# Attention's weights times values: seven of fifteen key tiles as three fp32r passes over high and low parts

## The reference

```python
scores = scale * np.matmul(q, k.transpose(0, 1, 3, 2))
scores = np.where(causal, -1000000000.0, scores)
a = np.exp(scores - scores.max(-1, keepdims=True))
a /= a.sum(-1, keepdims=True) + 1e-09
local = np.matmul(a, v)
mem_out = np.einsum('bhsd,bhde->bhse', phi(q), M_prev) / mem_norm
out = g * mem_out + (1 - g) * local
```

## Time and profile before

| | |
|---|---|
| Median of 3 runs | 870.16 us (870.12 to 870.6) |
| The profiled execution's own time | 870.0 us |
| Its span in the profile | 868.3 us |
| PE busy | 855.3 us (99%) |
| PEld busy | 755.7 us (87%) |
| DVE, ACT, POOL busy | 492.5, 317.6, 257.3 us |
| Attention | from the start to about 255.7 us |

### The profile page before, as it was taken

One profiled execution on the slowest core, in us unless ns is written; L12 is line 12 of the kernel. 1 busy time (PEld: TensorE's weight loads), 2 busy tenths in 40 slices (PEclk: granted clock), 3 DMA queues, 4 the chain that ended last, 5 costly groups with the idle time before them and its releaser, 6 DMA issues.

```text
span 868.3 us, 13401 instructions
## 1 busy us (share of the span) xinstructions
PE 855.3 (99%) x4966; PEld 755.7 (87%) x4966; DVE 492.5 (57%) x1036; ACT 317.6 (37%) x572; POOL 257.3 (30%) x371
## 2 busy tenths in 40 slices
PE   8999999999999999999999999999999999999998
PEld 7899999999888888888888889999998888888886
DVE  7766666666548865433443344344757655656664
ACT  6656566565432223222322222232243323232322
POOL 5656656565569992000000000000600000000000
PEclk9999999999999999999999999999999999999999
DMA  8665757564403322000000000000210000000000
GB/s 148 149 139 124 162 126 157 131 151 97 118 25 103 112 89 62 1 1 0 1 1 1 0 1 1 1 1 1 89 57 13 12 25 25 24 24 24 13 24 36
DMA packets 86359, 49.27 MB, mean 57 GB/s; under 512 B 65056, under 2 KB 73248, under 8 KB 86304
## 3 DMA queue, kind: packets, MB, share of 16 engines
q1 hardware_dynamic: 83760, 47.94, 22.8%
q10 hardware_dynamic: 2544, 0.59, 0.4%
HBM read 27.28 MB, written 4.72 MB: 37 GB/s over the span
## 4 chain that ended last, share of the span: by engine, by line
PE 89%; DVE 7%; issue 2%; ACT 1%; POOL 0%; POOLq 0%; ACTq 0%
PE ps_h L1265 8%; PE ps_h L1267 8%; PE ps_h L1266 8%; PE ps_y L1280 7%; PE ps_y L1282 7%; PE ps_y L1281 7%; PE ps_v L631 7%; PE ps_hid L1541 4%; PE ps_r L1570 4%; PE ps_s L546 4%; PE ps_hid L1543 4%; PE ps_hid L1542 4%; PE ps_r L1572 4%; PE ps_r L1571 4%; DVE spent L948 3%
## 5 line engine op out<-in xcount | busy, mean ns | idle before, releaser
L1384 DVE TENSOR_TENSOR xT<-xT 128x512 f32<-128x512 f32 (+1 forms) x80 | 60.3, 754 | 133.7 <-ACT xT L1340 133.7
L1265 PE MATMUL ps_h<-x_hi,win 128*128 128x512 f32 (+1 forms) x320 | 117.7, 368 | 0.0
L1267 PE MATMUL ps_h<-x_hi,win 128*128 128x512 f32 (+1 forms) x320 | 117.5, 367 | 0.0
L1282 PE MATMUL ps_y<-g_hi,wout 128*128 128x512 f32 (+1 forms) x320 | 117.5, 367 | 0.0
L1281 PE MATMUL ps_y<-g_lo,wout 128*128 128x512 f32 (+1 forms) x320 | 117.5, 367 | 0.0
L1266 PE MATMUL ps_h<-x_lo,win 128*128 128x512 f32 (+1 forms) x320 | 117.5, 367 | 0.0
L1280 PE MATMUL ps_y<-g_hi,wout 128*128 128x512 f32 (+1 forms) x320 | 117.4, 367 | 0.0
L631 PE MATMUL ps_v<-v_raw,pT 128*128 128x65 f32 (+1 forms) x960 | 107.6, 254 | 1.2 <-DVE t_loc L1046 1.2
L631 PEld LDWEIGHTS ps_v<-v_raw,pT 128*128 128x128 f32 (+1 forms) x960 | 101.3, 173 | 6.9 <-issue 4.7
L948 DVE CUSTOM_DVE_ANT_0 spent<-ps_s,mask 128x576 f32<-128x576 f32 (+4 forms) x160 | 81.6, 539 | 42.4 <-PE ps_s L546 41.6
L767 ACT ACTIVATE pT<-ps_x 128x512 f32<-128x512 f32 (+3 forms) x128 | 64.1, 501 | 94.5 <-PE ps_x L613 93.6
(11 more groups left out here) (164 smaller groups left out, 1685.7 us busy)
## 6 DMA issues: line engine op xcount, KB each, us to landing
stacked<-cut SPq DMA_DIRECT2D x56, 288.0 KB, 5.2
out<-res SPq DMA_DIRECT2D x18, 256.0 KB, 2.0
v_raw<-in_v SPq DMA_DIRECT2D x32, 128.0 KB, 3.2
stage<-in_moe_w_in SPq DMA_DIRECT2D x16, 256.0 KB, 2.7
stage<-in_moe_w_out SPq DMA_DIRECT2D x16, 256.0 KB, 2.6
k_raw<-in_k SPq DMA_DIRECT2D x28, 128.0 KB, 2.5
q_raw<-in_q SPq DMA_DIRECT2D x28, 128.0 KB, 3.6
stage<-in_moe_w_in SPq DMA_DIRECT2D x4, 512.0 KB, 3.8
```

The lines of the kernel that those rows point to most:

```text
L1265: pe.matmul(out, hi, x_hi[:, k, 0:n], start=(k == 0), stop=False)
L1267: ins = pe.matmul(out, lo, x_hi[:, k, 0:n], start=False, stop=(k == KT - 1))
L1282: ins = pe.matmul(out, wout[:, f, LO, w], g_hi[:, r, 0:n], start=False, stop=(f == FT - 1))
L1384: dve.tensor_tensor(r, r, r, ALU.mult).then_inc(square_done, 1)
```

## The change

Of the fifteen products of weights and values of a head, the seven with key tile j = 0 or 1 and a full query tile (t < 4) are done as three fp32r passes: high weights times high values (66 columns), high weights times low values (64 columns), low weights times high values (66 columns). It applies from head 4 (`WHOLE`) to head 31; heads 0 to 3 stay as they were. For this

- ACT writes the high weights `p_hi` (`round_weights`, two instructions a head: 384 columns for j=1 and 512 for j=0),
- DVE writes the low weights `p_lo` (`low_weights`, 384 and 512 columns),
- POOL writes the high and low values `v_cut` of key tiles 0 and 1, once a pair (`cut_values`),
[...]
- PE does `cross(h, 1)` before the first products of head h-1 instead of behind them, and waits there for `p_lo` and `v_cut` too,
- some buffers shrink: `stacked` holds keys and queries of a head next to each other, `fT` and `K1` lose the padding to 640 columns, `t_mem` has two buffers and not three, `least` one, `spent` shares places. The last memory product of a pair has 64 queries instead of 128.

Core of the diff:

```diff
@@ tensor: weigh_values
+                if is_cut(h):
+                    pe.wait_ge(v_lo_done, p - DIRECT + 1)
+                    pe.wait_ge(weights_low, 2 * (h - WHOLE) + 2)
             for t in ts:
+                where = EVEN * t
                 for j in range(t + 1):
                     at, m = p_at[j] + P * (t - j), rows_of[t]
-                    ins = pe.matmul(ps_v[0:m, par, E1 * t:E1 * (t + 1)], pT[par][:, at:at + m],
+                    if is_cut(h) and j < 2 and t < FULL:
+                        part = halves[j].start + P * (t - j)
+                        high = p_hi[par][:, part:part + P]
+                        low = p_lo[par][:, part:part + P]
+                        values = v_cut[h // 2 % 2]
+                        pe.matmul(ps_v[:, par, where:where + EVEN], high, values[:, 0, j, par, :],
+                                  start=(t == 0), stop=False, skip_group_check=True)
+                        pe.matmul(ps_v[:, par, where:where + D], high, values[:, 1, j, par, 0:D],
+                                  start=False, stop=False, skip_group_check=True)
+                        ins = pe.matmul(ps_v[:, par, where:where + EVEN], low, values[:, 0, j, par, :],
+                                        start=False, stop=(j == t), skip_group_check=True)
+                        continue
+                    ins = pe.matmul(ps_v[0:m, par, where:where + E1], pT[par][:, at:at + m],
                                     v_raw[h // 2 % 3][:, j, par, :], start=(t == 0),
@@ tensor: steps
+                if here:
+                    cross(h, 1)
                 if behind:
                     weigh_values(h - 1, (0, 1))
                 if ahead:
                     second_rows(h + 2)
-                if here:
-                    cross(h, 1)
@@ scalar
+        def round_weights(h, j):
+            act.wait_ge(tri_done, h * NT + (1 if j == 1 else 4))
+            act.wait_ge(exped, h * NC + (1 if j == 1 else 3))
+            act.activation(p_hi[h % 2][:, halves[j]], weights_of(h, j), ACT.Copy).then_inc(weights_rounded, 1)
...
                     exp_weights(h, 1)
+                if is_cut(h):
+                    round_weights(h, 1)
...
                     exp_weights(h, 3)
-                    if aside:
-                        aside(3)
+                if is_cut(h):
+                    round_weights(h, 0)
+                if here and aside:
+                    aside(3)
@@ vector
+        def low_weights(h, j):
+            dve.wait_ge(weights_rounded, 2 * (h - WHOLE) + (1 if j == 1 else 2))
+            if h > WHOLE + 1:
+                dve.wait_ge(pv_done, h - 1)
+            dve.tensor_tensor(p_lo[h % 2][:, halves[j]], weights_of(h, j), p_hi[h % 2][:, halves[j]],
+                              ALU.subtract).then_inc(weights_low, 1)
...
+                if is_cut(h - 1):
+                    low_weights(h - 1, 0)
                 if ahead or is_head(h + 1):
                     first_rows(h + 2)
                 if ahead:
                     second_rows(h + 2)
+                if is_cut(h):
+                    low_weights(h, 1)
+                if ahead:
                     third_rows(h + 2)
@@ gpsimd
+        def cut_values(p):
+            both, half = v_raw[p % 3][:, 0:2, :, :], v_cut[p % 2]
+            pool.wait_ge(v_in[p % 3], 16 * Q_DMAS * (p // 3 + 1))
+            need(pool, pv_done, 2 * (p - 2) + 2)
+            pool.tensor_scalar(half[:, 0, :, :, 0:E1], both, 1.0, 1.0, ALU.mult, ALU.mult).then_inc(v_hi_done, 1)
+            pool.wait_ge(v_hi_done, p - DIRECT + 1)
+            pool.tensor_tensor(half[:, 1, :, :, 0:D], both[:, :, :, 0:D], half[:, 0, :, :, 0:D], ALU.subtract).then_inc(v_lo_done, 1)
```

More of the change, by code:

```diff
@@ L117, in attention @@
     SLOTS, LATE = 3, 4
-    Q_HI, Q_LO, K_HI = range(3)
+    K_HI, Q_HI, Q_LO = range(3)
     MEM = 172
@@ L148, in attention @@
                         for places in ((pT[0][:, 0:THREE], all_t_mem[:, 0:THREE]),
-                                       (pT[1][:, 0:THREE], all_t_mem[:, THREE:2 * THREE])))
+                                       (pT[1][:, 0:THREE], all_relu[:, 0:THREE])))
     rm, rl = sb("rm", [P, NT, 2]), sb("rl", [P, 2, NT])
+    halves = {1: slice(0, wide[1] - REST), 0: slice(wide[1] - REST, wide[1] - REST + wide[0] - REST)}
+    p_hi, p_lo = ([sb(f"p_{n}{s}", [P, halves[0].stop], F32R) for s in range(2)] for n in ("hi", "lo"))
+    v_cut = [sb(f"v_cut{s}", [P, 2, 2, 2, EVEN], F32R) for s in range(2)]
     beta_in, inv_gate, inv_rest = (sb(n, [P, H]) for n in ("beta_in", "inv_gate", "inv_rest"))
@@ L219, in words, with is_cut, weights_of, both @@
         return view.bitcast(F32)
+    def is_cut(h):
+        return WHOLE <= h < HEADS
+    def weights_of(h, j):
+        return pT[h % 2][:, p_at[j]:p_at[j] + wide[j] - REST]
+    def both(view):
+        return view.rearrange("p (two s) -> p two s", two=2)
     def stacks_sent(p):
@@ L321, in gpsimd @@
                            base=0, pattern=[[-1, P]], channel_multiplier=1).then_inc(built, 1)
[L322 to L326, removed]
+        pool.memset(words(stacked[:, :, 2 * S:S + W]), 0.0).then_inc(cleared, 1)
+        pool.memset(least[:, :], 0.0).then_inc(cleared, 1)
         for s in range(3):
@@ L418, in steps @@
                     features(pr + 1)
+                if not even and is_pair(pr + 1):
+                    cut_values(pr + 1)
         double(first_k[1], k_in[1])
@@ L536, in memory @@
             for t in range(NT):
-                ins = pe.matmul(ps_t[:, MEM * t:MEM * t + 2 * E1], fT[p % 2][:, P * t:P * (t + 1)],
+                m = rows_of[t]
+                ins = pe.matmul(ps_t[0:m, MEM * t:MEM * t + 2 * E1], fT[p % 2][:, P * t:P * t + m],
                                 mz[:, p, :], start=True, stop=True)
@@ L574, in first_rows @@
             if is_head(h - 1):
-                ins = pe.transpose(ps_s[:, NEG_AT:NEG_AT + P], least[(h - 1) % 2][:, :], ident[:, :])
+                ins = pe.transpose(ps_s[:, NEG_AT:NEG_AT + P], least[:, :], ident[:, :])
             ins.then_inc(scored, 1)
@@ L611, in cross @@
                 out = ps_x[0:rows_of[j], c % 2, at:at + hi - lo]
-                pe.matmul(out, stacked[:, a, 1, some], stacked[:, a, 0, lo:hi], start=True, stop=False)
+                pe.matmul(out, stacked[:, a, some], stacked[:, a, S + lo:S + hi], start=True, stop=False)
                 ins = pe.matmul(out, K1[0:kept, p % LATE, par, some], Q1[0:kept, p % SLOTS, par, lo:hi],
@@ L809, in put @@
                 act.wait_ge(kT_turned, p + 1)
-                place, source = stacked[MINE[half], to, 1, 0:S], keys_psum(p)[MINE[half], 0:S]
+                place, source = stacked[MINE[half], to, 0:S], keys_psum(p)[MINE[half], 0:S]
             elif what[:-1] == "k_moved":
                 act.wait_ge(swapped_turned, K_SWAPPED[p])
-                place, source = stacked[MINE[1 - half], to, 1, 0:S], \
+                place, source = stacked[MINE[1 - half], to, 0:S], \
                     ps_x[:, :, :].rearrange("p two n -> p (two n)")[MINE[1 - half], 0:S]
@@ L816, in put @@
                 act.wait_ge(qT_turned, p + 1)
-                place, source = stacked[MINE[0], to, 0, 0:S], ps_t[MINE[0], 0:S]
+                place, source = stacked[MINE[0], to, S:2 * S], ps_t[MINE[0], 0:S]
             elif what == "q_own1":
@@ L822, in put @@
                 act.wait_ge(swapped_turned, Q_SWAPPED[p])
-                place, source = stacked[MINE[0], to, 0, 0:S], swapped_psum(p)[MINE[0], 0:S]
+                place, source = stacked[MINE[0], to, S:2 * S], swapped_psum(p)[MINE[0], 0:S]
             else:
@@ L946, in row_maximum @@
             n, r = keys[t], min(P, S - P * t)
-            at, at_row = sum(keys[:t]), SHIFT[h % 2].start + t
+            at, at_row = SPENT_AT[t], SHIFT[h % 2].start + t
             return dve.tensor_tensor_reduce(spent[:, at:at + n], ps_s[:, S_AT[t]:S_AT[t] + n],
                                             mask[:, FULL * P + r - n:FULL * P + r], -1.0, HUGE,
-                                            ALU.add, ALU.min, least[h % 2][:, at_row:at_row + 1])
+                                            ALU.add, ALU.min, least[:, at_row:at_row + 1])
         def first_rows(h):
@@ L1035, in scale_local @@
             kt = place(p)[1]
-            got = ps_v[:, :, 0:NT * E1].rearrange("p two (t e) -> p two t e", e=E1)
+            got = ps_v[:, :, 0:NT * EVEN].rearrange("p two (t e) -> p two t e", e=EVEN)
             dve.wait_ge(pv_done, 2 * p + 2)
```

56 lines of the change are left out of this document (31 added, 25 removed).

## The result

The changed kernel takes 902.95 us, the median of four runs (897.95 to 903.34), against 870.38 (870.12 to 870.82) of the kernel before on the same chip: 1.036 times as long [1.0324, 1.0397]. It is slower, as forecast, but 9.7 us above the forecast and 4 above the range's upper end. Its mean granted clock, 1.0 before, was 0.989, 0.994, 0.987 and 0.987 in the four runs; the quickest of them, 897.95, is the one at 0.994.

The account below looks back on a forecast made before the run. PE's list, busy 99% at full clock, was taken to bound the kernel, weight loads setting the changed products' pace. 870.0 + 21.6 (loads) + 0 (odd step) + 1.5 (end of attention) = 893.1, as median 893.3 us; range 886.5 to 898.8.

Parts of the forecast that it names:

- 196 products, one load more each: Seven products a head, heads 4 to 31: three loads, 0.333 us, replace 0.223; +21.6 us (18.0 to 23.9).
- Order of PE, buffers: `cross(h, 1)` moved ahead shrinks PE's wait for the row maximum, at best 2.8 us back; smaller buffers cost about nothing.
- Waits for `p_lo` and other feeding: Odd steps: PE waits for `p_lo` only if DVE's subtraction is slowed; taken as 0, at worst 2.8 us more.
- Wait at the end of attention: Last head's products wait for `p_lo`, which stands behind the first MLP's four `x_lo` on DVE: +1.5 us (1.1 to 1.9).
- The step that failed: Opening step: PE, busy 99% at full clock, bounds the kernel; attention grows by PE's list and its new waits.
- The load as the price of a pass: Each fp32r pass in attention costs one weight load, 0.111 us, whatever its 66 or 64 columns need; three cost 0.333.
- Rival 1: Fast loads: the passes' loads come at 0.058 us, a product costs 0.174 instead of 0.223; 862 us; 3%.
- rival 2: One load serves the two passes with the same high weights, so a product keeps its old price; 871.7 us; 2%.
- rival 3: Passes come closer than loads, 0.09 us apart: +9.2 us, 881 us; 4%.
- The rule on fast loads: Loads of 128 columns and non-FP32 type speed up by themselves; fp32r could count, giving the sum the other sign.
- The wait in an odd step: PE's wait for DVE's row maximum: PE comes 0.92 us later, DVE 0.69; taken as 0, 2.8 us either way.
- rival 4: DVE sets the pace: 512-column subtractions take 1.11 us, PE waits 0.42 in each of 28 heads; +11.8, 905 us; 8%.

Follow-up runs that it names:

- e1: The changed kernel with every product of weights and values in fp32 again, no parts made or waited for; new order and buffers stay: 865.98 us.
- e8: e2 with the last head's `p_lo` put ahead of the fourth `x_lo` on DVE: 891.27 us.
- e2: The changed kernel with each pass's moving columns read twice (132, 128, 132), the second copy going to PSUM columns nobody reads: 896.87 us.
- e5: The changed kernel without the second pass (high weights times low values), so two fp32r loads a product: 880.83 us.
- e7: The changed kernel with `p_hi`, `p_lo` and `v_cut` made and waited for, but the seven products of each head left in fp32: 881.14 us.
- e4: The changed kernel with only heads 4 to 27 in three passes, heads 28 to 31 left in fp32: 886.55 us.
- e9: The changed kernel with the last head's `p_lo` ahead of the fourth `x_lo` on DVE, passes as they were: 900.22 us.
- e10: e7 with the last head's `p_lo` ahead of the fourth `x_lo` on DVE: 877.87 us.

## Why the prediction was wrong

The measured terms are below. The loads and the wait at the end are read from traces. The others are differences of medians, less these two where it says so; the column therefore adds up by construction. A term that compares runs of different groups is uncertain by about half a microsecond.

| Term | Predicted | Measured |
|---|---|---|
| 196 products, one load more each | +21.6 | +21.8 (196 x 0.111 from the loads) |
| Order of PE, buffers | 0 (with the next) | -4.4 (e1 against before) |
| Waits for `p_lo` and other feeding | 0 | +3.5 (e8 - e1 - 21.8) |
| Wait at the end of attention | +1.5 | +2.2 (2.63 in e2 less 0.44 in e8) |
| Clock behind that wait | none | +3.4 (e2 - e8 - 2.2) |
| Clock under the narrow passes | none | +6.1 (after - e2) |
| Sum over before | +23.1 | +32.6 |

**The step that failed** is the first one: "PE is busy 99% of the span at a granted clock of full speed". That was read from before and carried over to the changed kernel as if it were a property of the core. The last sentence of the prediction named the case (wrong "if the granted clock leaves full speed"), but no rival had it and no end of the range paid for it. It is worth 3.4 + 6.1 = 9.5 us of the 9.7 missed, about what the half-clock stretches of the two traces can cost: 20.5 / 2 = 10.2 in the changed kernel. Rows for a warning were there: the pace of these products was already that of their loads, and the change makes three load and matmul records of two, at about the same 65 columns for each load. The other misses (+0.2, -4.4, +3.5, +0.7) cancel, by luck.

**The load as the price of a pass** was right, in size too: 0.11 apart, 21.8 against 21.6. Rival 1 (862), rival 2 (871.7) and rival 3 (881) need closer loads or one for two passes; neither is in the trace, and e5 and e7 agree. The rule on fast loads that the prediction takes from the Trainium skill, TensorE: Matmul & The Clock Gate, section Weight-path perf modes — Fast Weight Load (FWL) and DoubleRow, isn't borne out for the fp32r loads here: they last 195 to 197 ns each, fp32 ones 191.

**The wait in an odd step** came out near its 0 because two terms nearly cancel, which is luck: -4.4 for the order and +3.5 for the feeding. The order alone gives 14.69 - 14.44 = 0.25 us a pair, and 4.4 in all, above the 2.8 I had as the best case. What DVE newly does takes most of it back: over e1 a pair of e8 (16.09) is 1.65 longer, of which 14 x 0.111 = 1.55 are loads, so 0.10 a pair or 1.4 us are waits; the other 2.1 of the 3.5 lie outside the steady pairs and were not taken apart. A pair of 16.13 us fits the forecast 16.2.

**DVE as the pace (rival 4, 905)** came near the time, and for the wrong reason. DVE has slack in every pair and PE none; its subtraction of 512 columns took 0.68 or 0.82 us and not 1.11 in the steady part. DVE's work was under-priced all the same, 3.6 us a pair against 2.5, as 384 columns took 0.68 and 1.45 and not 0.554; the slack took it. ACT and POOL came out as sized (0.63 and 0.52 us; 1.1 a pair against 1.3). That the nearest forecast number was that of a wrong mechanism shows why the time alone doesn't settle one.

**The end of attention** was right as a mechanism, with DVE's `p_lo` behind the `x_lo` as releaser, and too small: 2.2 against 1.5 (1.1 to 1.9). The last `x_lo` ended 1.79 us after its start, with 1.09 for `p_lo` behind it; a late `x_hi` of ACT, 1.27 us of waiting, came on top. The `x_lo` was priced at 0.69 to 1.11: POOL was cutting the MLP's weights beside it (L1281, to 277.90), and `x_lo` ended 0.55 us after that. What a wait there does to the clock behind it was not in the term.

**Open:** what amount of work on the array decides, and over what time; why the clock falls in some runs and not in others of the same kernel (e4 and e8, one of four each), which also leaves the first fall of 6.8 us partly to chance; and whether values as the stationary operand, fewer loads for the same products, would save the change. None was tried.

## What to carry to other kernels

Price a split product by its weight loads: three passes of 66 columns under a 128-column load cost three loads, 0.333 us against 0.223 for fp32, however few columns move. When a change adds matmuls that are shorter than their loads, give the fall of the granted clock a price of its own (here up to half the length of the stretch, 9 us in e9 against e8), above all where the wide matmuls run out. If it falls, widening the moving operand up to the load's pace was free here and held it in three of e8's four runs; a move that only fills a regular wait, as `cross(h, 1)` ahead of the products, is worth taking alone: 0.5% with nothing else changed.

## What the runs showed of the hardware

- The granted clock fell to half with PE busy 96% of the 10 us before (9.63 of 10.00), in stretches of 3.4 to 17.1 us in the changed kernel and e9. A busy PE in the profile doesn't keep it up; passes of 132 columns at the same 0.11 us did where 66 didn't.
- It fell too behind waits of 1.5 to 3.2 us, with ordinary fp32 products on both sides (e7, e10). That such a wait is the cause is shown by e2 against e8: 2.63 us and a fall, 0.44 us and none.
- An fp32r load of 128 columns costs what an fp32 one does (195 to 197 ns against 191, 0.11 apart), and a second pass with the same weights loads them again.
- How long DVE's subtraction from SBUF to SBUF takes goes by what POOL is doing when it begins. With POOL idle, `p_lo` of 384 columns took 0.55 us (at 250.68) and of 512 columns 0.68. All fourteen of 384 columns that began while POOL's `xq` (L416) ran took 1.43 to 1.57 us and ended 0.41 to 0.42 us after it; those of 512 columns beside POOL's `fT` (L382) took 0.82 and ended 0.55 after it; at the end of attention 1.09 and, in e2, 1.75.
